# Strassen's token split of the second FFN moved from inside a 512-token tile to two whole tiles

## The chip, the cores and the metric

One core of a Trainium2 chip runs the whole program. The metric is the device time of one execution in microseconds (us). The profile is that of one execution, taken by the hardware profiler.

## The reference, cut to what is computed

```python
out = chunked_attention(q, k, v, mem_k, mem_v)   # 4 x 8 heads x 768 x 64
x = out.transpose(0, 2, 1, 3).reshape(3072, 512)
# first FFN
h = x @ w_in1                    # 512 -> 2048
g = s * relu(h) ** 2 + b
x = g @ w_out1                   # 2048 -> 512
# second FFN, the part that is changed
h = x @ w_in2                    # 512 -> 2048
g = h / (1 + exp(-1.702 * h))
out = g @ w_out2                 # 2048 -> 512
```

All is float32 outside. Inside, each operand of a matmul is split in two float32r parts, hi (a rounded copy) and lo (the rest), and each product is three matmuls: hi\*hi, hi\*lo, lo\*hi.

## The kernel before

There is one instruction stream per engine, in an order written out by hand, tied by semaphores; SyncE (SP) issues the DMAs. The first 58% of the span is attention together with the first FFN, in seven token tiles (M0 = 7, the last four of 480 tokens). The change does not touch it but for the last of these tiles, beside which the operands of the second FFN are prepared.

The second FFN runs in six tiles of 512 tokens. Its first product, w_in2 transposed times x, is done by Strassen's algorithm with seven products in place of eight. The rows of hidden features are taken in pairs of 128-row blocks (PAIRS = 8 pairs to a tile, so 48 turns `q`), the 512 input features in two halves of 256, and the tokens of a tile in two halves of 256 (HALF). One turn is seven products (`product`, L844 to L878), each of six matmuls with 256 columns: two of 128 input features, by three for hi and lo. Each goes to one of four PSUM banks. The seven weight sums (A11 to S4) of a pair are made once, for all eight pairs, and stay in `weights` for the whole stage; the seven token sums (B11 to T4) are made once per tile.

VectorE (DVE) puts the products together (`add_u2`, `add_u4`, `add_c12`, `add_c11`, `add_u3`, `add_c22`, `add_c21`, L1333 to L1366, each 128x256 from a PSUM bank and an SBUF tile). The four quadrants c11, c12 (even row block, two token halves) and c21, c22 (odd row block) form `h_even` and `h_odd`, each 128x512. ScalarE (ACT) copies the first product out (`keep_a11b11` L1080) and computes the sigmoids (`sigmoid_even` L1087, `sigmoid_odd` L1093); DVE multiplies (`gate_even` L1370, `gate_odd` L1374); ACT writes the hi part (`split_g2_hi` L1098) and DVE the lo part (`split_g2_lo` L1378) of what the second product eats.

The second product (`second_piece`, L813) takes one 128-row block f of the hidden features of one tile: four pieces (128 tokens each), each three matmuls with 512 columns, summed over f = 0 to 15 in the four banks `acc`. TensorE (PE) has the pieces of the pair before between the seven products: product, piece, product, piece, and at the end two pieces on end (L917 to L934). w_out2 comes anew for each tile, one 128-row block at a time: DMA (L449), hi by ACT (`split_w_out2_hi` L1055), lo by GpSimd (POOL, `split_w_out2_lo` L573) into a ring of four places.

Also beside this: `sum_rows` (POOL, L580 to L586) makes the weight sums of a pair, `split_rows_hi` (ACT, L1061) and `split_rows_lo` (DVE, L1324) split them, in one part of 128x1024 and one of 128x768; `sum_x2` (POOL, L591 to L598), `split_x2_hi` (ACT, L1074) and `split_x2_lo` (DVE, L1331) do the same with the tokens. `copy_result` (ACT L1109, DVE L1390) empties the four `acc` banks. Six of the eight weight pairs are made beside the last tile of the first FFN (steps of `ROWS_STEPS`), two in the second stage.

What a product waits for: the first of a turn for c11 of the turn before (and, in the first tile, for the weights of its pair), the second for u3, the third for c22, the fourth for c21, all of the turn before; the sixth for u2 and the seventh for c12 of its own turn. A second piece waits for hi and lo of its row block and for its w_out2 parts, and at f = 0 for the copies of the bank that it starts anew.

## Time and profile before

| what | value |
|---|---|
| three executions, median (lowest to highest) | 1205.45 us (1204.02 to 1214.04) |
| the profiled execution, its own time | 1205.65 us |
| its span in the profile | 1203.8 us |
| mean granted TensorE clock | 0.999 |
| PE busy / weight load busy | 99% / 89% |
| DVE / ACT / POOL busy | 63% / 55% / 30% |

The own time of an execution holds about 1.9 us around the span. A busy share is over the whole span; matmuls are pipelined and a recorded matmul is longer than the distance to the next one, so the cost of a matmul is read from the starts of successive ones. An instruction of DVE or ACT is likewise recorded somewhat longer than it keeps its engine from the next. "L876" is line 876 of the kernel before.

### The profile page before, as it was taken

To read this page: it belongs to the slowest core of one execution; us is meant where nothing else is said; L and a number is where in the kernel's file an instruction comes from. 1 tells how busy PE (TensorE), PEld (TensorE's weight loads), DVE (VectorE), ACT (ScalarE), POOL (GpSimd) and SP (SyncE) were. 2 spreads that over 40 slices of the span, in tenths; PEclk is the share of its full clock that TensorE was granted. 3 is DMA by queue.
4 is the path that set the end of the run, shared out by engine and by line. 5 is a ranking of instruction groups with operands and counts; after the bars stand their busy time and mean duration, and the time that the engine had idled before them with its cause. 6 is when DMAs were issued, how large, how long until landed. Compare 5 with 4: busy or idle time off the path is not lost. (4 is left out here: it accounts for less than half of the span.)

```text
span 1203.8 us, 21708 instructions
## 1 busy us (share of the span) xinstructions
PE 1190.3 (99%) x7224; PEld 1075.9 (89%) x7224; DVE 763.1 (63%) x2307; ACT 656.5 (55%) x1897; POOL 365.4 (30%) x364
## 2 busy tenths in 40 slices
PE   8899999999999999999999999999999999999998
PEld 5799999999888888888888889999999999999997
DVE  6788766777666666676536566655655656656554
ACT  6788666777666666666534444434433434444333
POOL 3775212222121121212015432422424224224221
PEclk9999999999999999999999999999999999999999
DMA  6752311321311311130021231231321311411211
GB/s 139 166 141 72 75 32 40 65 45 40 60 40 34 70 37 40 25 74 17 2 96 60 64 128 53 56 121 36 104 72 53 124 53 36 131 45 53 88 53 54
DMA packets 135637, 81.10 MB, mean 67 GB/s; under 512 B 95079, under 2 KB 115047, under 8 KB 135527
## 3 DMA queue, kind: packets, MB, share of 16 engines
q1 hardware_dynamic: 134304, 79.48, 25.2%
q8 instruction: 60, 0.98, 0.3%
q14 instruction: 50, 0.41, 0.1%
q10 hardware_dynamic: 1223, 0.23, 0.1%
HBM read 67.11 MB, written 12.58 MB: 66 GB/s over the span
## 5 line engine op out<-in xcount | busy, mean ns | idle before, releaser
L876 PEld LDWEIGHTS psum<-arena,weights 128*128 128x128 f32 x2016 | 285.6, 188 | 30.1 <-DVE arena_raw L1347 0.9
L808 PE MATMUL psum<-arena,weights 128*128 128x480 f32 (+1 forms) x1344 | 305.2, 366 | 0.2 <-DVE ffn L1311 0.2
L876 PE MATMUL psum<-arena,weights 128*128 128x256 f32 x2016 | 293.4, 281 | 0.5 <-DVE arena_raw L1347 0.5
L834 PE MATMUL psum<-g_hi,weights 128*128 128x480 f32 (+1 forms) x896 | 259.0, 363 | 0.1
L808 PEld LDWEIGHTS psum<-arena,weights 128*128 128x128 f32 x1344 | 237.8, 188 | 18.9 <-DVE ffn L1311 0.4
L832 PE MATMUL psum<-weights,g_hi 128*128 128x512 f32 x768 | 242.0, 396 | 0.1
L573 POOL TENSOR_TENSOR weights<-ffn,weights 128x512 fp32r<-128x512 f32 x94 | 129.4, 1396 | 327.8 <-ACT weights L1055 327.8
L834 PEld LDWEIGHTS psum<-g_hi,weights 128*128 128x128 f32 x896 | 164.5, 188 | 13.8 <-DVE g_lo L1317 0.4
L618 POOL TENSOR_TENSOR arena_raw<-arena_raw,small 96x256 f32<-96x256 f32 x96 | 58.6, 610 | 370.9 <-DVE small L1275 370.9
L834 PE MATMUL psum<-g_lo,weights 128*128 128x480 f32 (+1 forms) x448 | 163.4, 365 | 0.0
L832 PE MATMUL psum<-weights,g_lo 128*128 128x512 f32 x384 | 149.4, 389 | 0.0
L1255 DVE TENSOR_TENSOR arena<-psum,arena 128x96 fp32r<-128x96 f32 x336 | 83.2, 275 | 86.3 <-ACT arena L987 83.9
L832 PEld LDWEIGHTS psum<-weights,g_hi 128*128 128x128 f32 x768 | 122.3, 190 | 5.2 <-DVE g_lo L1378 0.3
L1087 ACT ACTIVATE arena_raw<-arena_raw 128x512 f32<-128x512 f32 x48 | 30.3, 632 | 164.2 <-issue 155.5
L992 ACT ACTIVATE arena_raw<-arena_raw,small 96x128 f32<-96x128 f32 x224 | 87.7, 392 | 35.1 <-DVE small L1264 34.9
L1317 DVE SCALAR_TENSOR_TENSOR g_lo<-ffn,columns,g_hi 128x480 fp32r<-128x480 f32 (+1 forms) x112 | 84.9, 758 | 29.1 <-ACT g_hi L1039 27.8
L1039 ACT ACTIVATE g_hi<-ffn,columns 128x480 fp32r<-128x480 f32 (+1 forms) x112 | 73.8, 659 | 45.2 <-PE psum L834 30.9
L1010 ACT ACTIVATE arena<-psum 64x96 fp32r<-64x96 f32 x224 | 54.7, 244 | 74.9 <-PE psum L751 70.5
L834 PEld LDWEIGHTS psum<-g_lo,weights 128*128 128x128 f32 x448 | 84.2, 188 | 6.4
L1378 DVE TENSOR_TENSOR g_lo<-arena_raw,g_hi 128x512 fp32r<-128x512 f32 x96 | 68.1, 710 | 33.9 <-ACT g_hi L1098 33.3
L832 PEld LDWEIGHTS psum<-weights,g_lo 128*128 128x128 f32 x384 | 72.2, 188 | 16.0
L1311 DVE SCALAR_TENSOR_TENSOR ffn<-psum,columns,ffn 128x480 f32<-128x480 f32 (+1 forms) x112 | 75.2, 671 | 15.3 <-ACT ffn L1031 10.9
(102 smaller groups left out, 1602.5 us busy)
## 6 DMA issues: line engine op xcount, KB each, us to landing
ffn<-in_moe_w_out_dram SPq DMA_DIRECT2D x94, 256.0 KB, 2.8
arena_raw<-in_k_dram SPq DMA_DIRECT2D x31, 240.0 KB
arena_raw<-in_v_dram SPq DMA_DIRECT2D x30, 240.0 KB
arena_raw<-x_scratch SPq DMA_DIRECT2D x6, 1024.0 KB, 5.6
arena_raw<-in_q_dram SPq DMA_DIRECT2D x31, 192.0 KB
out_dram<-result SPq DMA_DIRECT2D x5, 1024.0 KB, 4.5
result<-in_moe_w_out_dram SPq DMA_DIRECT2D x18, 256.0 KB, 3.0
result<-in_moe_w_in_dram SPq DMA_DIRECT2D x16, 256.0 KB, 3.1
```

The source lines that it names most:

```text
L573: nc.gpsimd.tensor_tensor(lo, w_out_raw(k), hi.bitcast(F32), ALU.subtract).then_inc(w_out2_ready, 1)
L618: nc.gpsimd.tensor_tensor(probs[:, n % 2, :, :], probs[:, n % 2, :, :], inv_total[:, n % 2, :].unsqueeze(2).to_broadcast([QT, 2, P]), ALU.mult
L808: last = nc.tensor.matmul(dst, w[:, kt * P:(kt + 1) * P], x, start=(kt + i == 0), stop=(kt == KT - 1 and i == 2))
L832: last = nc.tensor.matmul(acc[c][:, :], g[:, f % 2, piece], w, start=start, stop=stop)
L834: last = nc.tensor.matmul(acc[c][:, 0:n], w[:, piece], g[:, f % 2, 0:n], start=start, stop=stop)
L876: last = nc.tensor.matmul(bank_of[bank][:, 0:HALF], w[:, k * P:(k + 1) * P], x[:, k, :], start=(k + t == 0), stop=(k == 1 and t == 2))
L992: nc.scalar.activation(probs[:, n % 2, h, :], probs[:, n % 2, h, :], ACT.Exp, scale=-1.0, bias=exp_bias[:, n % 2, h:h + 1], accum_out=tota ...
L1039: nc.scalar.activation(g_hi[:, f % 2, 0:n], gated[:, 0:n], ACT.Identity, bias=b_col[:, 0:1]).then_inc(g_hi_done, 1)
L1255: last = nc.vector.tensor_tensor(qk_lo[parts, n % 2, cols], bank_qk[parts, source], qk_hi[parts, n % 2, cols].bitcast(F32), ALU.subtract)
L1311: nc.vector.scalar_tensor_tensor(out=gated[:, 0:n], in0=hid[f % 2][:, 0:n], scalar=s_col[:, 0:1], in1=nonlin[:, 0:n], op0=ALU.mult, op1=AL ...
L1317: nc.vector.scalar_tensor_tensor(out=g_lo[:, f % 2, 0:n], in0=gated[:, 0:n], scalar=b_col[:, 0:1], in1=g_hi[:, f % 2, 0:n].bitcast(F32), o ...
L1378: nc.vector.tensor_tensor(g_lo[:, e, :], (h_even, h_odd)[e], g_hi[:, e, :].bitcast(F32), ALU.subtract).then_inc(g_ready, 1)
```

## The change

A turn now covers two whole 512-token tiles, so that each of Strassen's products has 512 columns in place of 256. The second FFN has three blocks (BLOCKS = 3) of two tiles, 24 turns in place of 48. Of the four quadrants, c12 and c22 are those of the block's first tile (the "now" tile) and are used at once, as before; c11 and c21 are those of its second tile (the "later" tile), and are gated in place and kept in SBUF in float32 (`stored(f)`, 16 tiles of 128x512). After the eight turns of a block, PE has a stretch of second products alone: the last two row blocks of the now tile, and 14 of the later tile; its last two go between the products of the next block's first turn.

To make room, the weight sums do not stay: w_in2 is loaded, summed and split in each of the 24 turns, into two places in turn. The order of the token sums and who makes them change (T1 and T3 by POOL, T2 and T4 by DVE). For the later tile's row blocks, DVE makes the lo part of w_out2 in place of POOL. The raw tiles of w_out2 and the g tiles have four places in place of two.

The core of the diff:

```diff
-        def x2_parts(i, t):
+        def x2_parts(t):
+            pair, half = divmod(X2_ORDER.index(t), 2)
+            both = weights[:, pair, half * 2048:(half + 1) * 2048].rearrange("p (a k t) -> p a k t", a=2, k=2)
+        def rows_part(q, low, a):
+            first = (low * 7 + a) * HALF
+            return weights[:, 4 + q % 2, first:first + HALF]
+        def stored(f):
+            return weights_raw[:, 6 + f // 8, f % 8 * BT:(f % 8 + 1) * BT]
...
# SP
             def load_w_out2(k):
+                if k >= RING:
+                    sp.wait_ge(*w_out2_parts_made(k - RING))
-            def load_rows(p):
+            def load_rows(q):
+                p = q % PAIRS
+                if q:
+                    sp.wait_ge(rows_ready, q)
...
+            load_rows(1)
+            for s2 in range(BLOCKS):
+                for r in range(PAIRS):
+                    pair = PAIRS * s2 + r
+                    load_w_out2(turn(s2, 0, 2 * r + 2))
+                    load_w_out2(turn(s2, 0, 2 * r + 3))
+                    if r == 1:
+                        store_result(M0 + 2 * s2 - 1)
+                    if pair + 2 < PAIRS * BLOCKS:
+                        load_rows(pair + 2)
+                    if r == 2 and s2 + 1 < BLOCKS:
+                        load_x2(s2 + 1)
+                for f in range(NF):
+                    if turn(s2, 1, f + 2) < NF * 2 * BLOCKS:
+                        load_w_out2(turn(s2, 1, f + 2))
+                    if f == 2:
+                        store_result(M0 + 2 * s2)
...
# POOL
+            sum_rows(1)
+            for s2 in range(BLOCKS):
+                for r in range(PAIRS):
+                    q = PAIRS * s2 + r
+                    if q:
+                        split_w_out2_lo(turn(s2, 0, 2 * r))
+                        split_w_out2_lo(turn(s2, 0, 2 * r + 1))
+                    if r == 4 and s2 + 1 < BLOCKS:
+                        sum_x2(s2 + 1)
+                    if q + 2 < PAIRS * BLOCKS:
+                        sum_rows(q + 2)
...
# PE
-                        last = nc.tensor.matmul(bank_of[bank][:, 0:HALF], w[:, k * P:(k + 1) * P], x[:, k, :],
+                        last = nc.tensor.matmul(bank_of[bank][:, :], w[:, k * P:(k + 1) * P], x[:, k, :],
...
-            for q in range(PAIRS * M2):
+            for s2 in range(BLOCKS):
+                for r in range(PAIRS):
+                    q = PAIRS * s2 + r
+                    mm, f = (M0 + 2 * s2, 2 * r - 2) if r else (M0 + 2 * s2 - 1, NF - 2)
...
+                second_product(M0 + 2 * s2, NF - 2)
+                second_product(M0 + 2 * s2, NF - 1)
+                for f in range(NF - 2):
+                    second_product(M0 + 2 * s2 + 1, f)
...
# ACT
+            for s2 in range(BLOCKS):
+                for r in range(PAIRS):
+                    pair = PAIRS * s2 + r
+                    if r:
+                        split_now_hi(pair - 1, 1)
+                        sigmoid_c21(pair - 1)
+                    keep_a11b11(pair)
+                    if r == 1:
+                        copy_result(M0 + 2 * s2 - 1, 2)
+                    if pair:
+                        split_w_out2_hi(turn(s2, 0, 2 * r))
+                        split_w_out2_hi(turn(s2, 0, 2 * r + 1))
+                    if pair + 1 < PAIRS * BLOCKS:
+                        split_rows_hi(pair + 1)
+                    sigmoid_c12(pair)
+                    split_now_hi(pair, 0)
+                    sigmoid_c11(pair)
+                    if r == 0:
+                        copy_result(M0 + 2 * s2 - 1, 0)
+                    sigmoid_c22(pair)
+                split_now_hi(PAIRS * s2 + PAIRS - 1, 1)
+                sigmoid_c21(PAIRS * s2 + PAIRS - 1)
+                for f in range(NF):
+                    split_w_out2_hi(turn(s2, 1, f))
+                    split_later_hi(s2, f)
+                    if f == 2:
+                        copy_result(M0 + 2 * s2, 0)
+                        copy_result(M0 + 2 * s2, 2)
+                    if f in X2_HI and s2 + 1 < BLOCKS:
+                        split_x2_hi(s2 + 1, X2_HI[f])
...
# DVE
+            for s2 in range(BLOCKS):
+                for r in range(PAIRS):
+                    q = PAIRS * s2 + r
+                    if r:
+                        gate_c22(q - 1)
+                        split_g2_lo(turn(s2, 0, 2 * r - 1), h_odd)
+                        gate_c21(q - 1)
+                    if r == 1:
+                        copy_result(M0 + 2 * s2 - 1, 3)
+                    add_u2(q)
+                    if q + 1 < PAIRS * BLOCKS:
+                        split_rows_lo(q + 1)
+                    add_u4(q)
+                    add_c12(q)
+                    gate_c12(q)
+                    add_c11(q)
+                    split_g2_lo(turn(s2, 0, 2 * r), h_even)
+                    gate_c11(q)
+                    add_u3(q)
+                    add_c22(q)
+                    if r == 0:
+                        copy_result(M0 + 2 * s2 - 1, 1)
+                    add_c21(q)
+                gate_c22(PAIRS * s2 + PAIRS - 1)
+                split_g2_lo(turn(s2, 0, NF - 1), h_odd)
+                gate_c21(PAIRS * s2 + PAIRS - 1)
+                for f in range(NF):
+                    split_w_out2_lo(turn(s2, 1, f))
+                    split_g2_lo(turn(s2, 1, f), stored(f))
+                    if f in (1, 2):
+                        copy_result(M0 + 2 * s2, 2 * f - 1)
+                    if s2 + 1 < BLOCKS:
+                        if f in X2_LO:
+                            split_x2_lo(s2 + 1, X2_LO[f])
+                        if f in X2_SUMS:
+                            sum_x2(s2 + 1, X2_SUMS[f])
```

Beside the last tile of the first FFN, the new kernel makes the seven token sums of block 0 (each part 128x1024, twice the size of before), the weight sums of pair 0, and the first two row blocks of w_out2. Then `split_rows_hi(q)` waits until all seven products of turn q - 2 are done.

## Rows read from the trace of the kernel before

**Rows 1.** The page: busy time by engine, the chain's shares by line.

```profile
PE 1190.3 (99%) x7224; PEld 1075.9 (89%) x7224; DVE 763.1 (63%) x2307; ACT 656.5 (55%) x1897; POOL 365.4 (30%) x364
...
PE psum L832 22%; PE psum L876 19%; DVE weights L1324 0%; ACT weights L1061 0%; ACT arena_raw L1087 0%; DVE g_lo L1378 0%; ACT result L1109 0%; ACT weights L1055 0%; DVE arena_raw L1358 0%; DVE arena_raw L1362 0%; DVE arena_raw L1347 0%; DVE arena_raw L1370 0%
```

**Rows 2.** Busy time of stretches: first FFN's last tile, second FFN's steady part.

```profile
607.00:688.00 81.00, 81.00 (x375) 70.02 (x374) 44.51 (x52) 34.83 (x54) 29.86 (x30) 1.00 0.24 75
719.42:1193.72 474.30, 474.30 (x2971) 427.67 (x2971) 275.06 (x543) 198.39 (x362) 152.49 (x110) 1.00 0.23 70
```

**Rows 3.** Timeline of PE: start us, us, engine, line, what, xcount.

```profile
688.13 0.88 PE L876 MATMUL psum<-arena,weights 128*128 128x256 f32 x6
...
904.05 0.87 PE L876 MATMUL psum<-arena,weights 128*128 128x256 f32 x6
904.76 0.63 PE L832 MATMUL psum<-weights,g_hi 128*128 128x512 f32 x2
...
908.98 0.63 PE L832 MATMUL psum<-weights,g_hi 128*128 128x512 f32 x2
...
910.36 0.88 PE L876 MATMUL psum<-arena,weights 128*128 128x256 f32 x6
...
1194.94 0.61 PE L832 MATMUL psum<-weights,g_hi 128*128 128x512 f32 x2
...
1200.16 0.39 PE L832 MATMUL psum<-weights,g_lo 128*128 128x512 f32 x1
```

**Rows 4.** Timeline of DVE and ACT; in brackets idle before, and releaser.

```profile
783.06 0.69 DVE L1390 COPY result<-psum 128x512 f32<-128x512 f32 x1
...
907.53 0.69 DVE L1370 TENSOR_TENSOR arena_raw<-arena_raw 128x512 f32<-128x512 f32 x1 [0.75 <-ACT arena_raw L1087]
908.14 0.42 DVE L1358 TENSOR_TENSOR arena_raw<-psum,arena_raw 128x256 f32<-128x256 f32 x1
908.60 0.42 DVE L1362 TENSOR_TENSOR arena_raw<-psum,arena_raw 128x256 f32<-128x256 f32 x1
...
911.56 0.62 ACT L1098 ACTIVATE g_hi<-arena_raw 128x512 fp32r<-128x512 f32 x1
912.08 0.62 ACT L1074 ACTIVATE arena<-arena_raw 128x512 fp32r<-128x512 f32 x1
```

**Rows 5.** Timeline of ACT and DVE: one pair's weight sums are split.

```profile
681.98 1.79 ACT L1061 ACTIVATE weights<-arena_raw 128x1024 fp32r<-128x1024 f32 x2 [3.31 <-POOL arena_raw L586]
...
683.08 2.09 DVE L1324 TENSOR_TENSOR weights<-arena_raw,weights 128x1024 fp32r<-128x1024 f32 x2 [3.35 <-ACT weights L1061]
...
685.09 0.71 DVE L1311 SCALAR_TENSOR_TENSOR ffn<-psum,columns,ffn 128x480 f32<-128x480 f32 x1
```

**Rows 6.** Timeline of POOL beside DVE, where both read SBUF.

```profile
702.65 2.56 POOL L573 TENSOR_TENSOR weights<-ffn,weights 128x512 fp32r<-128x512 f32 x2 [9.77 <-ACT weights L1055]
...
704.08 3.08 DVE L1324 TENSOR_TENSOR weights<-arena_raw,weights 128x1024 fp32r<-128x1024 f32 x2 [0.44 <-ACT weights L1061]
...
713.65 0.74 POOL L586 TENSOR_TENSOR arena_raw<-arena_raw 128x256 f32<-128x256 f32 x1
713.66 1.27 DVE L1378 TENSOR_TENSOR g_lo<-arena_raw,g_hi 128x512 fp32r<-128x512 f32 x1 [0.70 <-ACT g_hi L1098]
714.35 3.00 POOL L573 TENSOR_TENSOR weights<-ffn,weights 128x512 fp32r<-128x512 f32 x2
...
715.38 0.42 DVE L1342 TENSOR_TENSOR arena_raw<-psum,arena_raw 128x256 f32<-128x256 f32 x1
```

**Rows 7.** A weight load and its use; POOL's 128x512 group after 690 us.

```profile
707.18 0.93 SPq L460 DMA_DIRECT2D arena_raw<-in_moe_w_in_dram  x2
710.86 0.74 POOL L580 TENSOR_TENSOR arena_raw<-arena_raw 128x256 f32<-128x256 f32 x1 [5.66 <-DMA arena_raw<-in_moe_w_in_dram]
L591 POOL TENSOR_TENSOR arena_raw<-arena_raw 128x512 f32<-128x512 f32 x5 | 6.5, 1291 | 0.0
```

**Rows 8.** PE's timeline: a stall in this stage.

```profile
707.54 0.98 PE L876 MATMUL psum<-arena,weights 128*128 128x256 f32 x6 [0.46 <-DVE arena_raw L1347]
```

More of the change, by code:

```diff
@@ L46 @@
 USES = {t: 1 + [x[1] for x in PRODUCTS].index(t) for t in range(7)}
+X2_ORDER = (B22, B21, B11, T1, T3, T2, T4)
+X2_NTH = {t: 1 + X2_ORDER.index(t) for t in range(7)}
 PAIRS = NF // 2
@@ L198, in bass_chunked_attention_two_ffn @@
-        h_even = raw_area(XSLOT + 9216, 512)
-        h_odd = raw_area(XSLOT + 9728, 512)
-        nonlin2 = raw_area(XSLOT + 10240, 512)
-        kept_a11b11, u2, u3 = (raw_area(3072 + i * HALF, HALF) for i in range(3))
-        def rows_raw(p):
-            return raw_area(0 if p >= PAIRS - 2 else XSLOT + 9216, 7 * HALF)
-        def w_out_raw(k):
-            return result[:, k * DM:(k + 1) * DM] if k < 2 else ffn[:, k % 2, :]
-        def raw_of(t):
-            k, half = {B11: (0, 0), T1: (0, 0), T3: (0, 1), B21: (2, 0), T4: (2, 0), B22: (2, 1), T2: (2, 1)}[t]
-            return x2_raw[:, k:k + 2, half * HALF:(half + 1) * HALF]
@@ L216, in rows_lo, with rows_parts @@
-        def rows_lo(p, a):
-            return weights[:, p, LOW + a * HALF:LOW + (a + 1) * HALF]
-        def rows_hi(p, a):
-            return weights[:, p, HIGH + a * HALF:HIGH + (a + 1) * HALF]
-        def ring(k):
-            return (weights[:, k % RING * 2 + a, REST:REST + DM] for a in range(2))
+        def rows_part(q, low, a):
+            first = (low * 7 + a) * HALF
+            return weights[:, 4 + q % 2, first:first + HALF]
+        def rows_parts(q, low):
+            return weights[:, 4 + q % 2, low * 7 * HALF:(low + 1) * 7 * HALF]
@@ new lines, in ring @@
+        def ring(k):
+            slot = k % RING
+            if slot < 2:
+                return (weights[:, 3, 2048 + (2 * slot + a) * DM:2048 + (2 * slot + a + 1) * DM] for a in range(2))
+            if slot == 2:
+                return (weights[:, 4 + a, 14 * HALF:14 * HALF + DM] for a in range(2))
+            return (area(2560 + a * DM, DM) for a in range(2))
+        def stored(f):
+            return weights_raw[:, 6 + f // 8, f % 8 * BT:(f % 8 + 1) * BT]
+        kept_a11b11, u2, u3, h_even, h_odd = (raw_area(i * BT, BT) for i in range(5))
@@ L227, in bass_chunked_attention_two_ffn, with raw_of @@
+        def raw_of(i, t):
+            if t == T1:
+                return (ffn if i else nonlin2.rearrange("p (k t) -> p k t", k=2))[:, :, :]
+            k, half = {B11: (0, 1), T3: (0, 0), B21: (2, 1), T4: (2, 1), B22: (2, 0), T2: (2, 0)}[t]
+            return x2_raw[:, k:k + 2, half * BT:(half + 1) * BT]
         q_raw = attn[0:QT, 0:2 * DM].rearrange("p (a c) -> p a c", a=2)
@@ L464, in load_x2 @@
             def load_x2(i):
-                if i == 0:
-                    sp.wait_ge(hid_ready, NF * (M0 - 1) + 1)
-                else:
+                if i:
                     sp.wait_ge(x2_ready, 7 * i)
-                first = start_of(M0 + i)
-                last = first + size_of(M0 + i)
+                first, last = 2 * BT * i, 2 * BT * (i + 1)
                 sp.wait_ge(result_stored, 16 * (1 + min(m for m in range(M0) if start_of(m) + size_of(m) >= last)))
@@ L1060, in split_rows_hi @@
                 for these in (slice(0, 4 * HALF), slice(4 * HALF, 7 * HALF)):
-                    nc.scalar.activation(weights[:, p, HIGH:REST][:, these], rows_raw(p)[:, these], ACT.Copy
+                    nc.scalar.activation(rows_parts(q, 0)[:, these], rows_raw[:, these], ACT.Copy
                                          ).then_inc(rows_hi_done, 1)
             def split_x2_hi(i, t):
-                if t < T2:
+                if t in (T1, T3):
+                    act.wait_ge(x2_first_summed, 2 * i + (1 if t == T1 else 2))
+                elif t in (T2, T4):
+                    act.wait_ge(x2_last_summed, 2 * i + (1 if t == T2 else 2))
+                else:
```

397 lines of the change are left out of this document (186 added, 211 removed).

## The prediction

> **What bounds the kernel now.** I read the page's busy times and chain first, then busy time by stretch, then the timelines of PE, of DVE and ACT, and of POOL beside DVE. The page puts the whole chain of the second stage on PE: the second product (L832) and Strassen's products (L876) hold 22% and 19% of the span, everything else next to nothing [rows 1]. By stretch, PE is busy 474.30 us of 474.30 in the steady part of this stage, and 81.00 of 81.00 beside the last tile of the first FFN, while DVE has 275 us and ACT 198 us of the 474 [rows 2]. So PE's own pace is the bound, and the question is what the change does to that pace, and whether the other engines, which get longer instructions with fewer gaps, can still follow.
>
> PE's pace comes from starts in its timeline. A product of six 256-column matmuls takes 904.05 to 904.76, 0.71 us, 0.1185 each; two pieces of together six 512-column matmuls take 908.98 to 910.36, 1.38 us, 0.2305 each; in the last stretch, of second products alone, 23 matmuls take 1194.94 to 1200.16, 0.227 each [rows 3]. The stage begins at 688.13 and its last matmul ends at 1200.55 [rows 3]: 512.4 us. Its floor is 2016 x 0.1185 + 1152 x 0.2305 + 24 of 480 columns (5.2, taken by width) = 509.6; the rest is small stalls like the 0.46 us at 707.54 [rows 8] and rounding.
>
> **The change part by part.** *PE.* 2016 matmuls of 256 columns become 24 x 7 x 6 = 1008 of 512. The trace has no 512-column matmul inside a product; the nearest rows give 0.227 to 0.2305 [rows 3]. I take 0.229: 230.8 us, where the half-size ones cost 2016 x 0.1185 = 238.9. Half of the second product's 1152 matmuls, some 600, now run without products between them, as in the last stretch, at about 0.2275: 136.5 us; the other 552 at 0.231 cost 127.5; plus 5.2. PE's new floor is 500.0 us, 12.4 below the 512.4 of now (bounds 497.7 to 503.8, with 0.227 or 0.2305 throughout). So twice the width halves the number of matmuls but hardly their total time: the most that can be won is about 1%.
>
> A rule bears on this. The trace has 0.1185 us for 256 columns, where the columns at 2.4 GHz (granted clock 1.00 [rows 2]) would take 0.107, so some 0.012 us per matmul goes with the count. The Trainium skill, TensorE: Matmul & The Clock Gate, section "Wait — 56ns, not 53.3ns?", states a fixed 2.5 ns on top of the columns; by it the products would shrink by only 2.6 us in place of 8.1. The trace's distances are larger, and the sum goes by them.
>
> *DVE and ACT in a turn.* A turn of PE is now 42 x 0.229 + 24 x 0.2308 = 15.16 us. The durations at twice the width: a 128x512 instruction of DVE that reads PSUM takes 0.69 us, as does one on SBUF, and the next starts 0.61 later; one that needs the result of the one ahead starts 0.04 after that one's end (908.14 + 0.42 to 908.60) [rows 4], so 0.73 after its start. ACT takes 0.62 and lets the next start after 0.52 [rows 4]. The two hi parts of a pair's weight sums take 1.79 us on ACT (about 1.05 for the wider), the two lo parts keep DVE from 683.08 to 685.09, 2.02 [rows 5]; these now come in every turn. Along the new order they close a ring, each step ending later than the step of PE that it also waits for:
> hi of the wider part, 1.09 with handoff; both lo parts on DVE, 2.02 (u4 stands behind them in DVE's queue); u4 0.73, c12 0.73, sigmoid 0.67, gate 0.60, c11 0.73, sigmoid 0.67, gate 0.60, u3 0.73, c22 0.73, sigmoid 0.67, gate 0.73: 7.59; then on ACT hi of the row block 0.52, sigmoid of c21 0.54, the copy of A11B11 0.52 and two hi parts of w_out2 1.04, all ahead of the next weight sums in its queue: 2.62. Sum 13.32 us, 1.84 below PE's turn.
>
> *The port.* POOL's share grows: the four weight sums (4 x 0.74 [rows 6], with gaps 3.2 us) in each of 24 turns, beside two lo parts of w_out2 (2.56 [rows 6]), so 5.8 us in 15.2. Where both work on SBUF, the one that comes second waits for the other's whole instruction: the weights' lo parts took 3.08 in place of 2.09 when they began 0.1 us into POOL's second instruction (702.65 + 1.28), and a 0.69 us instruction took 1.27 next to a POOL one begun 0.01 earlier; then POOL's pair took 3.00 in place of 2.56, and DVE's addition out of PSUM at 715.38 was not held [rows 6]. The Trainium skill, SBUF — State Buffer, section "Who interferes with whom", has this as an exclusive lock for the whole instruction, taken where DVE reads both inputs from SBUF; the trace agrees, and it speaks against the change.
> In the new order the w_out2 parts of POOL start just when the weights' hi parts are done: DVE finds the port held by the first or second of them, 1.1 us. The gate of c11 falls among the weight sums of the next pair, whose load takes 3.7 us from issue to use (707.18 to 710.86 [rows 7]) after the lo parts: 0.73, and the gate of c22 0.23. With these 2.06 us the ring is 15.38, against 15.16 of PE. Per turn that costs 0.2 us, and only once the slack with which a block starts (DVE has caught up in the stretch without products) is used up. The port waits can be anything from 0 to about 4 a turn, so the ring is 13.3 to 17.3; I take 15.4.
>
> *sum_x2 on POOL*, at turn 4 of blocks 0 and 1, is two instructions of twice 128x512. One 128x512 takes 1.29 [rows 7], so 2.45 each. They stand behind the w_out2 parts, and the second half of DVE's lo parts finds the port taken: it starts 2.45 us late, u4 and c12 with it, and the seventh product waits for c12. Walking the queues of this turn with the durations above, c12 is there at 14.1 us of the turn where PE asks at 12.1: a stall of 2.0 us in block 0. Turns 5 to 7 have nothing to spare and add 0.2 to 0.5 each, 1.0 together. In block 1 the same walk begins with more slack: 0.4, then 0.9. Block 2 has no such sum and I get no stall in its turns.
>
> *The end of a block* (0 and 1). The now tile's last row block, c22 of turn 7, is wanted after the two last pieces and one second product, 15.2 + 2.7 = 18.0 us into the turn. u3 comes at 16.6 as DVE is late by then; c22, c21, sigmoid, gate (with port), hi and lo take till 21.0: 3.0 us. The bank copies of ACT, which stand behind hi parts held up by this, come 0.7 late. Twice 3.7 = 7.4. In block 2, DVE is on time (u3 at 12) and both vanish. All stalls: 3.0 + 1.3 + 7.4 + 0.5 of smaller ones = 12.2 us.
>
> *The stretch without products.* 14 second products of 12 x 0.2275 = 2.73 us. DVE has 1.2 us for each (w_out2 lo and g lo), plus 9 instructions of 1.15 for the next tokens: 30 us of 44; ACT 1.04 each plus seven of 1.05. Four places in each ring let both run ahead. Cost 0; POOL is nearly idle here, so no port waits. *Loads.* 16 more loads of a pair's weights (512 KB each) go past SP in each turn with 10 us to spare, on DMA queues that moved 70 GB/s on average [rows 2]; cost 0, cover the 15 us turn. *Beside the last tile of the first FFN*, five weight pairs fewer and token parts of twice the size on engines that have 45 and 35 us of work in 81 [rows 2]; cost 0, up to 2 us if a POOL instruction holds a g part. *The kernel's end* is unchanged.
>
> **Sum.** 500.0 + 12.2 = 512.2 us for the stage, 0.2 less than the 512.4 of now. The profiled execution took 1205.65 us, 0.2 above the median of the three runs: 1205.4, and as a median 1205.
>
> **Rivals.** *PE stays the bound.* If the port waits are about 1 us a turn, the ring stays under 15.16 and sum_x2 and the block ends cost 2 to 3 us in all: stage 502.5, time 1195.7. For it: DVE lost nothing where it came first, as its 0.7 us instructions mostly do now, and 0.2 us of the ring decide. Against it: the order puts POOL's parts just ahead of DVE's largest instructions, and two POOL instructions on end leave no gap.
> *The ring decides, slower.* If each of some nine handoffs of the ring between engines takes 0.08 more than the 0.04 that I took, the ring is 16.1; with 3.5 us of port waits a turn it is 16.8. With 16.1, the same walk gives 26.8 us of stalls, a stage of 526.8, time 1220: 2 us for each 0.1 beyond 15.4. It is slower by over 1% from a ring of about 16.0 on. For it: ring and PE are within 2%, everything in the ring is in series, and DVE's busy share rises from 58% to over 70% in the turns. Against it: it takes handoffs of three times the length, or a third more port time.
> *That nothing of the width is won*, because 512 columns in a product cost 0.237: stage 520, time 1213, inside the forecast's side; the rows at 0.2305 speak against it.
>
> **How the numbers follow.** My forecast, a ring within 0.4 us of PE's turn, 0.64; PE bound 0.17; the ring decides 0.17; no width gain 0.02. A measurement of this kernel tells about 1% (12 us) from no change. Under 1193.4 only the lower half of the PE case lies, with a floor near 498: 0.10. Over 1217.5 lies most of the slower case: 0.15. The rest, 0.75, is within 1%. The range of 8 in 10 is 1195 (PE bound) to 1219 (ring of 16.1).
>
> **What would show it.** Right: product matmuls 0.229 apart; PE idle at the seventh product of turns 4 to 7 waiting for c12 (DVE), 2.0 us once and tenths after; 3 us at the second last row block of the now tile in blocks 0 and 1 waiting for g lo; block 2's turns at 15.2; DVE's weight lo parts over 3 us beside POOL. Wrong: turns of 15.2 everywhere, or 16 and more from turn 2 on, or PE waiting for weight loads or w_out2 parts, or the stage's floor off 500 by more than 4.

## The result and the profile after

The changed kernel takes 1190.44 us (median of five, 1190.09 to 1192.11) against 1205.45: a ratio of 0.9879, 95% interval 0.9848 to 0.9911. That is faster by 1.2%. The forecast was 1205 with a range of 1195 to 1219, and it was wrong; the rival "PE stays the bound" (1195.7) is what happened, though with port waits of 1.6 us a turn and not the "about 1" that it asked for, and even its time was 5 us too long.

The page of the kernel after, its busy times and its chain, which answer to [rows 1] (products are L910 now, second products L867):

```profile
PE 1172.3 (99%) x6216; PEld 1023.1 (86%) x6216; DVE 835.5 (70%) x2204; ACT 674.9 (57%) x1884; POOL 335.2 (28%) x362
...
PE 82%; DVE 6%; ACT 6%; issue 4%; POOL 1%; ACTq 0%; DVEq 0%; POOLq 0%
PE psum L869 21%; PE psum L842 20%; PE psum L867 18%; PE psum L910 13%; PE psum L785 3%; PE psum L809 3%; PE psum L796 2%; DVE weights L1404 1%; PE psum L773 1%; PE psum L772 1%; ACT weights L1101 1%; ACT weights L1111 1%; ACT arena_raw L1033 1%; PE psum L707 1%; ACT arena L1020 1%
```

PE is still the chain, and DVE has gone from 63% to 70%. The 6% of DVE and of ACT are no sign of the change, though. The chain of before was followed back only to 703 us, that of after through attention too; and in a second execution of this kernel (after_again, below), whose stage is as long to 0.05 us, PE holds 490 of the chain's last 500 us, where it holds 371 here. How short waits are shared out on the chain differs from one execution to the next, so what PE loses is read from the distances between its matmuls. Busy time by stretch, second stage (685.14 to 1185), answers to [rows 2]:

```profile
685.14:1185.00 499.86, 496.23 (x2185) 409.43 (x2183) 378.99 (x487) 237.50 (x385) 150.27 (x138) 1.00 0.30 93
```

PE is idle for 3.6 us by this count. From the stage's first matmul (685.14) to its last matmul's start (1184.69) it is 499.55 us; before it was 688.13 to 1200.16, 512.03. So 12.5 us came from the stage. The stage also began 3.0 us earlier, and that has nothing to do with the change. The first 60 us of four executions show it, in this order: after, before, before run once more, after run once more. The columns are PE, weight load, DVE, ACT and POOL busy, granted clock, DMA share, GB/s:

```profile
0.00:60.00 60.00, 52.95 (x406) 41.73 (x406) 42.34 (x196) 43.58 (x161) 35.05 (x39) 1.00 0.78 158
```
```profile
0.00:60.00 60.00, 52.30 (x387) 40.47 (x388) 40.70 (x189) 40.70 (x151) 31.90 (x36) 0.97 0.70 152
```
```profile
0.00:60.00 60.00, 53.20 (x404) 42.10 (x405) 42.28 (x195) 43.36 (x160) 34.75 (x38) 1.00 0.72 157
```
```profile
0.00:60.00 60.00, 53.67 (x337) 41.42 (x338) 34.56 (x163) 33.88 (x126) 26.77 (x31) 0.74 0.61 132
```

The granted clock at the start was 1.00, 0.97, 1.00 and 0.74, and the stage then began at 685.1, 688.1, 685.5 and 696.8 us. In the last of these the clock was at its lower level (1.2 GHz) from about 15 to 45 us, while PE was busy; the row is after run once more:

```profile
20.00:25.00 5.00, 5.00 (x31) 3.87 (x32) 2.94 (x14) 3.09 (x14) 2.27 (x2) 0.50 0.24 54
```

One program differs from itself by nearly 12 us before the stage begins, so in what follows kernels are compared by the stage alone, from its first matmul to the start of its last.

PE's timeline, turn 4 of block 0 and the end of block 0, answers to [rows 3]. The last column is the idle time before and what ended it:

```profile
746.93 1.52 PE L910 MATMUL psum<-weights 128*128 128x512 f32 x6
748.29 0.84 PE L867 MATMUL psum<-weights,arena 128*128 128x512 f32 x3
748.97 1.52 PE L910 MATMUL psum<-weights 128*128 128x512 f32 x6
...
804.73 2.88 PE L867 MATMUL psum<-weights,arena 128*128 128x512 f32 x12
808.88 3.02 PE L867 MATMUL psum<-arena 128*128 128x512 f32 x12 [1.26 <-DVE arena L1486]
812.37 0.70 PE L867 MATMUL psum<-weights,g_hi 128*128 128x512 f32 x2 [0.47 <-ACT result L1184]
```

A product takes 1.36 us and a piece 0.68: nine matmuls in 2.04 us, 0.2267 each, products and pieces alike. No turn of PE has a stall: the starts of all turns stand 14.96 us apart (66 x 0.2267), the first of the stage 14.88. What stalls there are stand at the ends of blocks 0 and 1, by the distances between matmuls 1.42 and 0.63 in block 0, 1.62 and 0.60 in block 1, and 0.19 in each block for the matmul just behind them: 4.66 us. PE's floor in the stage is then 494.9 us.

DVE and POOL in turn 4 of block 0 (from 744.89), where the forecast had its 2.0 us, answer to [rows 5, 6]:

```profile
749.40 5.28 DVE L1404 TENSOR_TENSOR weights<-arena_raw,weights 128x1024 fp32r<-128x1024 f32 x2 [0.22 <-ACT weights L1111]
754.60 0.68 DVE L1440 TENSOR_TENSOR arena_raw<-psum,arena_raw 128x512 f32<-128x512 f32 x1
755.38 0.69 DVE L1445 TENSOR_TENSOR arena_raw<-psum,arena_raw 128x512 f32<-128x512 f32 x1
```
```profile
747.97 2.55 POOL L606 TENSOR_TENSOR weights<-arena_raw,weights 128x512 fp32r<-128x512 f32 x2 [2.81 <-ACT weights L1101]
750.48 3.38 POOL L627 TENSOR_TENSOR ffn<-arena_raw 128x1024 f32<-128x1024 f32 x1
```

Both lo parts meet POOL, as forecast: first its w_out2 lo part, then the first x2 sum, and 2.08 us of work (the same pair in turn 0, alone) takes 5.28. But c12 (L1445) is written at 756.07, 11.2 us into the turn. The forecast had 14.1, and PE asks at 12.2.

### The profile page after: what moved, and what is told of

It reads as the page before. It is cut to its first block, busy times and chain, and to the rows that moved or that the text cites. A ratio compares the mean times of both kernels' runs of the same rounds, so it can differ in the third digit from the quotient of the medians.

```text
span 1188.3 us, 19471 instructions
## 1 busy us (share of the span) xinstructions
PE 1172.3 (99%) x6216; PEld 1023.1 (86%) x6216; DVE 835.5 (70%) x2204; ACT 674.9 (57%) x1884; POOL 335.2 (28%) x362
## 4 chain that ended last, share of the span: by engine, by line
PE 82%; DVE 6%; ACT 6%; issue 4%; POOL 1%; ACTq 0%; DVEq 0%; POOLq 0%
PE psum L869 21%; PE psum L842 20%; PE psum L867 18%; PE psum L910 13%; PE psum L785 3%; PE psum L809 3%; PE psum L796 2%; DVE weights L1404 1%; PE psum L773 1%; PE psum L772 1%; ACT weights L1101 1%; ACT weights L1111 1%; ACT arena_raw L1033 1%; PE psum L707 1%; ACT arena L1020 1%
## 5 line engine op out<-in xcount | busy, mean ns | idle before, releaser
L910 PE MATMUL psum<-weights 128*128 128x512 f32 x1008 | 255.9, 389 | 0.0
L842 PEld LDWEIGHTS psum<-arena,weights 128*128 128x128 f32 x1344 | 237.7, 188 | 18.9 <-DVE ffn L1391 0.4
L910 PEld LDWEIGHTS psum<-weights 128*128 128x128 f32 x1008 | 189.2, 188 | 39.2
L867 PE MATMUL psum<-weights,g_hi 128*128 128x512 f32 x384 | 118.4, 390 | 0.9 <-ACT result L1184 0.9
L606 POOL TENSOR_TENSOR weights<-arena_raw,weights 128x512 fp32r<-128x512 f32 x36 | 46.3, 1298 | 217.8 <-ACT weights L1101 217.8
L1072 ACT ACTIVATE ffn<-psum 128x480 f32<-128x480 f32 (+1 forms) x112 | 60.0, 536 | 52.1 <-PE psum L842 51.7
L867 PEld LDWEIGHTS psum<-weights,g_hi 128*128 128x128 f32 x384 | 71.9, 188 | 16.6 <-DVE g_lo L1486 1.7
L1020 ACT ACTIVATE arena<-psum 128x96 fp32r<-128x96 f32 x336 | 75.6, 259 | 16.9 <-PE psum L773 14.1
L1404 DVE TENSOR_TENSOR weights<-arena_raw,weights 128x1024 fp32r<-128x1024 f32 (+1 forms) x48 | 76.3, 1628 | 12.1 <-ACT weights L1111 12.1
L1344 DVE CUSTOM_DVE_ANT_0 arena_raw<-psum,masks 96x128 f32<-96x128 f32 x224 | 55.4, 283 | 36.0 <-ACT arena L1051 35.6
```

What stands on the lines that cost most here:

```text
L842: last = nc.tensor.matmul(dst, w[:, kt * P:(kt + 1) * P], x, start=(kt + i == 0), stop=(kt == KT - 1 and i == 2))
L867: last = nc.tensor.matmul(acc[c][:, :], g[:, piece], w, start=start, stop=stop)
L910: last = nc.tensor.matmul(bank_of[bank][:, :], w[:, k * P:(k + 1) * P], x[:, k, :], start=(k + t == 0), stop=(k == 1 and t == 2))
L1020: last = nc.scalar.activation(qk_hi[parts, n % 2, cols], bank_qk[parts, source], ACT.Copy)
L1072: nc.scalar.activation(nonlin[:, 0:n], hid[f % 2][:, 0:n], ACT.Relu).then_inc(nonlin_done, 1)
L1404: last = nc.vector.tensor_tensor(rows_parts(q, 1)[:, these], rows_raw[:, these], rows_parts(q, 0)[:, these].bitcast(F32), ALU.subtract)
```

## The experiments

Edits are against the kernel after, unless said. "Lag" is how far into PE's turn ACT begins the hi parts of the next pair's weight sums (L1111); in the kernel after it is 3.67 in turn 1, falls by 0.08 a turn to 3.43 in turn 4, jumps to 5.57 in turn 5 behind the x2 sums and is 5.40 in turn 7.

**before_again.** The kernel before, once more.

> The kernel before, unchanged, for a second profile. The changed kernel was 3.0 us ahead already when the second FFN began (685.1 us in place of 688.1), all of it gained in the first 49 us, where both programs are the same. If that lead is an accident of one profile (loads that land sooner or later), this profile starts the second FFN somewhere between 684 and 689 us and its stage takes 512.4 us again. If the change itself gives the lead, it starts at 688.1 again.

Measured: 1202.96 us. The stage begins at 685.53 (688.13 in the profile of before, 685.14 after) and takes 512.03 us, the same to 0.01. So the stage's lengths can be compared to hundredths, and 2.6 of the 3.0 us before the stage are the start's own.

**after_again.** The kernel after, once more. Expected was a stage of 499.55 us again, within 0.1, and 1190 to 1192 us for executions with a mean clock of 1.000; the rival was that the change itself makes the start 3.0 us faster.

Measured: 1191.68 us as a median of six (ratio 0.9897, 0.9856 to 0.9938); the three with a mean clock of 1.000 took 1190.6 to 1191.3, the profiled one with 0.987 took 1201.78. Its stage is 499.60 us, with the same stalls at the ends of blocks (1.51 and 0.60, 1.58 and 0.64).

**split256.** Each product as twelve matmuls of 256 columns, `half` being the first and then the second 256, all else as changed:

```diff
-                        last = nc.tensor.matmul(bank_of[bank][:, :], w[:, k * P:(k + 1) * P], x[:, k, :],
+                            last = nc.tensor.matmul(bank_of[bank][:, half], w[:, k * P:(k + 1) * P], x[:, k, half],
```

> The changed kernel with each 512-column matmul of a product issued as two of 256 columns; everything else is as changed. Theory pace: what was won is TensorE's time per column. 256-column matmuls stand 0.118 us apart, 512-column ones 0.2267, and the second product's matmuls between short ones 0.2305. A turn is then 84 x 0.118 + 24 x 0.2305 = 15.47 us in place of 14.96, 12.2 us more over 24 turns, of which up to 4 come back since the other engines now have slack: 1198 to 1203 us. Theory structure: what was won is fewer and longer steps and fewer waits: then this stays at 1190 to 1192 us.

Measured: 1206.23 us (ratio 0.9993, 0.9955 to 1.0032); stage 509.29 us without a single stall, turns 15.58. The median of the times says little: five of the ten executions had the low clock at the start (0.987 to 0.989; 1209.8 to 1211.7 us), the other five took 1199.9 to 1202.7.

```profile
731.96 1.59 PE L911 MATMUL psum<-weights 128*128 128x256 f32 x12
733.39 0.86 PE L867 MATMUL psum<-weights,arena 128*128 128x512 f32 x3
734.09 1.59 PE L911 MATMUL psum<-weights 128*128 128x256 f32 x12
```

Twelve halves take 1.43 us where six whole ones take 1.36, and three pieces 0.70 where they take 0.68. The gain is PE's own and comes from the width: without it the stage is 9.7 us longer, and against PE's floor of 494.9 the width gives 14.4, of which the stalls take 4.7. All the rest of the change gives 2.7 us (512.03 to 509.29). With a slower PE there are also no stalls.

**ladder.** Five of the six matmuls of each product cut to 64, 128, 192, 240, 256, 272, 320 and 416 columns in turns 0 to 7 of a block (this leaves out part of every product).

> The changed kernel with five of the six matmuls of each product cut to 64, 128, 192, 240, 256, 272, 320 and 416 columns in turns 0 to 7 of a block (so most of the hidden features are left out of the sums); the trace gives the distance of matmuls at each width. Theory issue: a matmul with its weight load cannot follow the last one sooner than some 0.118 us: distances stay at 0.118 from 64 to 256 columns, are 0.120 at 272 and 0.142 at 320, and the 512-column matmul after the short ones stands 0.233 from the next. Theory fixed cost: each matmul costs its columns at 2.4 GHz and about 0.012 us more: 0.039, 0.065, 0.092, 0.112, 0.118, 0.125, 0.145, 0.185.

Measured, the median distance from one such matmul to the next between neighbours of its own width: 111, 112, 113, 112 ns for 64 to 240 columns, then 120 (256), 125 (272), 147 (320), 189 (416), 216 (480, from the first FFN) and 227 (512). Two rows of turn 0:

```profile
686.69 0.86 PE L911 MATMUL psum<-weights 128*128 128x512 f32 x6
687.39 0.68 PE L869 MATMUL psum<-g_hi,weights 128*128 128x480 f32 x2
```

One matmul of 512 and five of 64 columns take 0.70 us, hardly less than six of 256 took before (0.71 [rows 3]): up to 240 columns a matmul between others as narrow costs 0.112 us, however narrow it is. Above, 256 and 512 columns fit one line of 0.0042 us per 10 columns and about 0.013 per matmul (0.120 and 0.227). The ladder gives no reading of the loop's own length, as the short turns let DVE and ACT fall behind.

**ring_plus.** Two more 128x256 copies on ACT in each turn, ahead of the w_out2 hi parts.

> The changed kernel with two more 128x256 copies on ScalarE in each turn (into a place that nothing reads), ahead of the two hi parts of w_out2. Theory ring: the ring of waits between ScalarE and VectorE takes 14.88 us in the changed kernel, 0.08 below TensorE's turn; with 0.56 more it is 15.44, which is what was predicted. c12 has 3.0 us to spare in turn 1, loses 0.48 a turn and 2.2 by sum_x2 in turn 4: stalls of 0.7 in turn 4, 0.5 in turns 5 to 7 and 1.1 more at the end of the block, 3.2 us in each of blocks 0 and 1, next to none in block 2: 6 to 7 us slower, 1197 us. Theory hidden: ScalarE is busy 57% and the copies cost nothing: 1190 to 1191 us.

Measured: 1197.49 us (ratio 0.9957, 0.9928 to 0.9987), stage 505.03, 5.5 us more. The copies keep ACT for 0.60 us, but the lag grows by only 0.23 a turn where it fell by 0.08: 0.31. The other 0.29 comes off the wait for the port, since the lo parts now begin later in POOL's instruction (the pair takes 2.77 us, not 3.08). Until late in turn 4 PE feels nothing; its first stall is at that turn's seventh product, 0.43 us in block 0 and 0.81 in block 1. From turn 5 the lag is 7.0 and stops there, and PE waits instead. Block 2, where the lag only gets to 5.9, has no stall. Of the 5.5 us, 1.6 are matmuls at 1.2 GHz behind the stall at the end of block 0. What PE waits for is what the forecast named, only later and less:

```profile
PE psum L869 <- DVE arena L1493: 4.6, 2, 2.3
PE psum L912 <- DVE arena_raw L1452: 0.5, 1, 0.5
PE psum L869 <- ACT result L1191: 0.5, 1, 0.5
```

**rows_first.** ACT makes the hi parts of the weight sums ahead of the two w_out2 hi parts:

```diff
                     keep_a11b11(pair)
...
+                    if pair + 1 < PAIRS * BLOCKS:
+                        split_rows_hi(pair + 1)
                     if pair:
                         split_w_out2_hi(turn(s2, 0, 2 * r))
                         split_w_out2_hi(turn(s2, 0, 2 * r + 1))
-                    if pair + 1 < PAIRS * BLOCKS:
-                        split_rows_hi(pair + 1)
```

> The new kernel with one move on ACT: the two hi parts of the sums' weight rows go ahead of the two w_out2 hi parts. Theory (the stalls that are left, 4.66 us at the ends of blocks 0 and 1, come from a lag of the loop over ACT and DVE behind TensorE of about 5.4 us in turns 5 to 7, of which POOL's two x2 sums give 2.2 in turn 4): the hi parts begin about 1.0 us earlier behind TensorE's turn (3.5 to 2.5 us), the first weight lo part begins before POOL's w_out2 lo part and takes 1.2 us in place of 2.21, so the lag in turns 5 to 7 falls from 5.5 to 3 or 4 and the stalls at the block ends go from 4.66 us to under 1; the stage from 499.6 to about 495.5, the time 4 us under the new kernel's. Rival 1 (the lag has nothing to do with it: the block ends stall by their own chain of now rows and bank copies): the stage stays at 499.6 within 0.5. Rival 2 (POOL takes the port between the two lo parts, so that the second takes 2.2 in place of the first): the loop gains 1.0 us at most, the stalls fall by half, the stage is about 497.5.

Measured: 1186.94 us (ratio to before 0.9846, 0.9812 to 0.9879), stage 495.01, 4.5 us less. The lag is 2.1 in all turns but 1 (2.7 to 3.0), 5 (4.8) and 6 (2.9), and the stalls are 0.2 us in the whole stage. Rival 2 is right about the port and wrong about the result:

```profile
721.86 3.18 DVE L1404 TENSOR_TENSOR weights<-arena_raw,weights 128x1024 fp32r<-128x1024 f32 x2
```
```profile
722.13 4.06 POOL L606 TENSOR_TENSOR weights<-arena_raw,weights 128x512 fp32r<-128x512 f32 x2 [4.50 <-ACT weights L1101]
```

DVE comes first this time (721.86, POOL 722.13), POOL gets the port between the two lo parts, and the pair takes 3.18 us, no less than before. Now POOL waits too (4.06 in place of 2.55), off any path. What was won is the 1.0 us of w_out2 parts on ACT, which no longer stand in the loop.

**sumx2_gap.** POOL's two x2 sums in turns 4 and 5, each behind the lo parts of its turn:

```diff
-                    if r == 4 and s2 + 1 < BLOCKS:
-                        sum_x2(s2 + 1)
+                    if r in (4, 5) and s2 + 1 < BLOCKS:
+                        pool.wait_ge(rows_ready, q + 2)
+                        sum_x2(s2 + 1, r - 4)
```

> The new kernel with POOL's two x2 sums put into turns 4 and 5, each after the lo parts of the weight rows, where DVE has short operations only. Theory (the x2 sums hold the port under a weight lo part, 5.28 us for the pair of lo parts in turn 4 in place of 3.1, and that lag of 2.2 us lasts to the block's end and is what stalls TensorE there): the lag of the hi parts in turns 5 to 7 stays under 4.2 us in place of 5.4 to 5.7, both stalls of 1.4 to 1.6 us on a g_lo row go, the stage comes to about 495.5 and the time 4 us under the new kernel's. Rival (an x2 sum in the gap delays u4, c12 or a gate by its own 2.5 us, and these are what TensorE's next product waits for): stalls of 1 to 2 us move into turns 4 and 5, and the stage stays within 1 us of 499.6.

Measured: 1193.36 us as a median of four executions (ratio 0.9884, 0.9831 to 0.9937), of which two had the low clock at the start (0.989; 1196.7 and 1197.5) and two not (1188.5 and 1190.0), so the times alone do not tell it from the kernel after; stage 496.90, 2.65 us less. No stall in a turn. In block 0 the lag is 4.5 in turn 7 and 0.64 us of stall on the g_lo row are left; in block 1 it is 3.84 and there is none. The 0.6 to 0.7 us for a bank copy stays in both. The pair of lo parts takes 3.08 in turn 4 too. The jump of 2.2 us was thus the first x2 sum under the lo parts; about 0.8 in two turns is what the sums cost in the gap (c12's gate 0.94 in place of 0.69, and the weight sums behind them).

**both.** Meant as both moves together, but as run it had the hi parts of the weight sums one place further ahead, in front of the copy of A11B11 too.

> Both moves together. Theory: the loop of ACT and DVE is about 1 us a turn shorter than TensorE's turn of 14.96 and carries no lag to the block's end, so TensorE never waits in the stage: stage 494.9 (499.55 less the 4.66 us of stalls), time 4.7 us under the new kernel's. Rival (the ends of blocks have a chain of their own): at least 1.2 us (2 x 0.6, the waits for a bank copy) stay, stage 496.1 or more.

Measured: 1210.77 us (ratio 1.0041, 1.0013 to 1.0070), stage 519.23: turns of 14.96 to 15.14 us up to turn 3, then 16.1 to 17.1, in block 2 as well, where no x2 sum runs. ACT's timeline:

```profile
717.44 1.78 ACT L1114 ACTIVATE weights<-arena_raw 128x1024 fp32r<-128x1024 f32 x2
719.13 0.58 ACT L1135 ACTIVATE arena_raw<-psum 128x512 f32<-128x512 f32 x1
719.60 1.14 ACT L1104 ACTIVATE weights<-arena_raw 128x512 fp32r<-128x512 f32 x2
```

and DVE's:

```profile
719.80 0.69 DVE L1437 TENSOR_TENSOR arena_raw<-psum,arena_raw 128x512 f32<-128x512 f32 x1 [1.46 <-ACT arena_raw L1135]
720.41 4.23 DVE L1407 TENSOR_TENSOR weights<-arena_raw,weights 128x1024 fp32r<-128x1024 f32 x2
```

u2 (L1437) now waits for the copy, which stands behind the hi parts; the lo parts stand behind u2, each of the two meets one of POOL's parts, and the pair takes 4.2 us. The loop is about 16.4 us long: this is the forecast's slower rival, made real by one more place in ACT's queue.

**both2.** The two moves as they were meant, hi parts behind the copy.

> The hi parts of the sums' weight rows ahead of the two w_out2 hi parts, and behind the copy of A11B11 this time, with POOL's x2 sums in turns 4 and 5. Theory (the order of the copy and the hi parts cost the 24 us of the kernel in which the hi parts were ahead of both: u3 waited for the copy, the lo parts came late and both of them then met POOL's w_out2 parts): every turn 14.96 us, no stalls, stage 494.9 to 495.1, time equal to rows_first (1186.94) within 1 us. Rival (POOL's wait for the lo parts in turns 4 and 5 is what cost it, since the loads of the weights stand behind POOL): turns of 16.4 us from turn 4 on again, stage over 515.

Measured: 1186.76 us (ratio to before 0.9839, 0.9794 to 0.9884), stage 495.02, all turns 14.96. The order of the copy and the hi parts was the cause. POOL's wait alone is not, and brings nothing on top of rows_first, as there was no stall left to take.

**rows_first_plus.** rows_first with the two extra copies of ring_plus.

> rows_first with the two extra 128x256 copies of ACT in each turn, which cost the new kernel 5.5 us (stage 505.0 against 499.55). Theory (with the hi parts first the loop is over 0.6 us a turn shorter than TensorE's turn, so it has room for the copies): turns 14.96 us, stalls under 0.5 us in all, stage 495.0 to 495.5. Rival (the loop is at balance there too and the order only shifted its phase): the lag grows by 0.3 us a turn again, stage 497 or more.

Measured: stage 495.03, stalls 0.26 us, lag 2.1 again (one execution, 1193.8 us with a clock of 0.993 and a stage that began only at 693.4). Copies that cost the changed kernel 5.5 us cost nothing here. This shows that their place matters, and not how much room the loop has: they now stand behind the hi parts of the weight sums, where ACT waits 3.9 us for DVE in rows_first. What room there is shows in rows_first itself, where the lag falls from 4.8 to 2.9 us from turn 5 to turn 6, in a turn whose lo parts met no POOL part (2.09 us), while in the kernel after it falls by 0.08.

**late_start.** Three extra 128x512 copies on ACT, each waited for, behind the first sigmoid of the stage.

> The new kernel with three extra 128x512 copies on ACT, each waited for, behind the first sigmoid of the stage: ACT and DVE start the stage 2.0 us later behind TensorE, once, as the prediction had them. Theory (the loop of ACT and DVE takes 14.88 us a turn, TensorE 14.96, so a lag is kept and hardly worked off; TensorE stalls once the rows' hi parts begin over 7.0 us into its turn, as they did with two more copies a turn): in block 0 the hi parts begin at 5.6 us in turns 1 to 4 and at 7.0 in turn 5, where TensorE stalls for about 0.5 us, and at the end of block 0 the wait for a g_lo row grows from 1.4 to about 2.7 us; block 1 and block 2 as in the new kernel. Stage 501.2 us (499.55 + 0.5 + 1.3), up to 503 if the wait at the block's end lets the granted clock fall for some matmuls, as in the run with two more copies. Rival (the lag at a block's end comes from POOL and the port alone, and a late start is caught up within the turns): the hi parts are back at 3.5 us by turn 4, stage 499.6.

Measured: 1193.59 us (ratio 0.9906, 0.9871 to 0.9942), stage 501.46. The copies took 1.95 us, of which 1.0 arrived in the lag: 4.69 in turn 1, 4.46 in turn 4, 6.42 in turn 5, 6.23 in turn 7. It is kept, as said, and block 1 is as in the kernel after. At the seventh product of turn 4 PE stalls 0.14 us, at the end of block 0 2.24 where it was 1.42, and then:

```profile
800.00:809.00 9.00, 9.00 (x41) 7.27 (x39) 8.02 (x11) 2.47 (x4) 3.38 (x4) 1.00 0.39 117
811.00:816.20 5.20, 4.95 (x15) 3.95 (x16) 5.20 (x10) 5.20 (x10) 0.00 (x0) 0.67 0.21 54
816.20:820.00 3.80, 3.80 (x18) 3.13 (x17) 3.42 (x5) 3.08 (x6) 0.00 (x0) 1.00 0.63 213
```

PE goes on at 811.25, and from 813 to 816 its matmuls stand 0.427 us apart (granted clock 0.67 over the stretch of 5.2 us, that is 1.2 GHz for part of it): 1.6 us more, beside which the 0.7 for the bank copy is gone. So the stage met its forecast of 501.2 in part by luck: the lag and the stalls came out smaller (4.7 and 6.4 us, 0.14 and 0.8 more, where 5.6 and 7.0, 0.5 and 1.3 were expected), and the clock made up for it.

## Why the prediction was wrong, by its steps

The forecast was 15 us too long (1205.4 against 1190.4). By the profiles: PE's floor 4.9 (495.1 with the last matmul itself, as the forecast counted), stalls 7.5, the start 3.0. So two steps failed. The price of a 512-column matmul was drawn up towards rows of before whose neighbours are narrow (0.229 for the products, 0.231 for half of the pieces), though the row with neighbours as wide gave 0.227; all cost 0.2267. And the walk of the queues had ACT and DVE too late behind PE: a ring longer than PE's turn, and c12 2.9 us too late, which made 12.2 us of stalls where 4.66 were measured. The kinds of wait, at the ends of blocks and at the port, were right.

*The base, 1205.65.* It came from an execution whose clock was 0.97 in its first 60 us, 2.6 us later at the stage than before_again. The text called it 0.2 above the median, which is true and hid it: executions of this program with a mean clock of 1.000 take 1202.5 to 1204.1.

*PE's floor: 500.0, measured 494.9.* Two terms were mis-sized. The product matmuls were taken at 0.229 and cost 0.2267 (2.3 us). The pieces were taken at 0.231 between products and 0.2275 apart from them, and also cost 0.2267 (2.8 us). The row behind 0.2305 [rows 3] was read as the price of a piece. It is the price of a piece behind short matmuls: in before_again the three matmuls of a piece that follows 256-column ones cost 233, 236 and 228 ns (medians), against 227 where their neighbours are as wide. This goes away when the product is widened. split256 shows it from the other side: it keeps the 256 columns, and the same 233, 236 and 228 ns behind them, but has half as many crossings from short to wide (168, not 336). Its second products are 4.0 us shorter than those of before (273.2 to 269.2): 2.9 for the crossings at 17 ns each, 0.2 for pieces on end, some 0.9 for the stalls that before has. Its products are 1.3 us longer (238.8 to 240.1), which leaves the 2.7. So the 12.5 us are: 1008 for 2016 product matmuls 10.3 (238.8 less 228.5), crossings 5.8 (336 x 17.3 ns) and 0.5 of the same kind in second pieces on end, a stall of before 0.5 [rows 8], less 4.66 of new stalls: 12.4. The rule of the Trainium skill (TensorE: Matmul & The Clock Gate, "Wait — 56ns, not 53.3ns?"), 2.5 ns on top of the columns, is further off than the text had it: 256 and 512 columns both give about 13 ns, and the products shrank by 10.3 us, not 2.6 (1008 fewer matmuls at 2.5 ns are 2.5).

*The ring, 15.38 against 15.16.* The ring without port was right: 14.88 measured, less port waits of 1.6, is 13.3, and the text had 13.32. The port waits were sized 2.06; in the turns the wide lo part takes 2.21 in place of 1.2 (1.0), the gate of c11 1.23 in place of 0.69 (0.54), the gate of c22 0.76 (0.07). So the ring was 0.5 us shorter and PE's turn 0.2 us shorter than thought, and the order of the two turned round: 14.88 under 14.96 instead of 15.38 over 15.16. The text had said that 0.2 us of the ring decide.

*Stall at turn 4 (2.0 and 1.0; 0.4 and 0.9).* Measured: none. The mechanism was there in full, the lo parts at 5.28 us and a lag 2.2 us longer to the end of the block, but c12 came 11.2 us into the turn, not 14.1. Of the 2.9 us, 0.3 a turn for three turns is the ring, which was to add 0.2 and took off 0.08. The other 2 us are a remainder. The expectation of late_start puts them down to the start of the stage, where the walk would have had ACT and DVE that much too late. The prediction does not print where its walk began, so what made up the 2 us is not shown; one candidate of 1.28 us is ACT's table load, which in the trace falls into a wait:

```profile
687.19 1.78 ACT L1111 ACTIVATE weights<-arena_raw 128x1024 fp32r<-128x1024 f32 x2
688.99 1.28 ACT L1138 ACT_TABLE_LOAD   x1
693.53 0.63 ACT L1138 ACTIVATE arena_raw<-arena_raw 128x512 f32<-128x512 f32 x1 [3.26 <-DVE arena_raw L1445]
```

In the kernel before it had come late, at 695.00, behind a wait of 5.58 us for DVE. late_start and ring_plus put a part of the lag back (1.0 and 1.6 us in turn 4), and the stall at the seventh product returned, with 0.14 and 0.43 us in block 0.

*The ends of blocks, 2 x 3.7.* Place and kind were right (g lo of the now tile first, then the bank copies), the size was not: 4.66 in all. The size follows the lag: with a lag of 3.84, 4.5, 5.40, 5.58 and 6.23 us in turn 7 the stall on the g lo row was 0, 0.53, 1.42, 1.62 and 2.24 us, one for one above some 4.0. At a lag of 7.0 (ring_plus) it was 2.45 and 2.43, half a microsecond under that line. A walk 2 us late at the stage's start can account for block 0 only: late_start changed block 0 and left block 1 as it was. What made block 1's 3.7 too large (2.4 measured) is not parted by any run; a ring thought 0.3 us a turn too long works in that direction.

*Block 2, the stretch without products, loads, the last tile of the first FFN: 0.* Right; PE has no stall of note in any. The stage starts at 685.14 in after and at 685.53 in before_again; variants that are the same as after up to there start it between 685.2 and 686.5 with the same start clock of 1.00, so no effect of what lies ahead, the five weight pairs fewer among it, can be told from that scatter.

*The port* was right as a mechanism, in the trace and in four experiments: the waits are for the whole of the other engine's instruction, and an instruction that comes later waits less, to the tenth (ring_plus). The Trainium skill says the first too (SBUF — State Buffer, "Who interferes with whom"): the lock is exclusive, and whoever issues first has the shared ports for the whole instruction.

*The chances.* "Faster by over 1%" stood at 0.10 since the floor's lower bound had been 497.7. That bound was added up wrongly: 2160 matmuls at 0.227, "throughout", and 5.2 are 495.5 us, and the upper one at 0.2305 is 503.1, not 503.8. The floor measured by the same count, 495.1, lies just under the right lower bound, which was a row of the trace of before: the 23 matmuls whose neighbours are all as wide [rows 3]. With 495.5 the case "PE stays the bound" would have reached down to about 1191 us with its 2 to 3 us of stalls, and the chance of over 1% would have been larger.

## What to carry to other kernels

The distance between matmuls belongs to a pair of neighbours, not to a line of code: before pricing a change of width, sort the distances by the width of the matmul ahead and look what the change does to the neighbours, too. Where two loops are within a few per cent of each other, a lag that one event leaves stays for the rest of the block; so ask what cheap work stands in the longer loop for no reason. One such move on ACT took 4.5 us off the stage here, and with one place more it was 20 us longer than it had been. And price the start of the profiled execution against a second one before its time is taken as the base.

## What was unexpected of the hardware

- The granted clock in the first 60 us, a mean over stretches at 2.4 and 1.2 GHz, was 1.00, 0.97, 0.86, 0.77 or 0.74 in the thirteen profiles, and the stage then began at 685.1 to 686.5, 687.8 to 688.1, 693.4, 695.2 or 696.8 to 696.9 us. It goes with nearly all the spread of the times: of the 17 executions of the kernel before that ran beside both, the 11 with a mean clock of 1.000 took 1202.7 to 1204.1 us, one with 0.998 took 1205.0, and the five with 0.987 to 0.993 took 1210.3 to 1214.3.
- Up to 240 columns a float32r matmul with weights of its own costs 0.112 us between others of its width; 256 columns cost 0.120. Six halves of a product were thus close to where halving brings nothing.
- Matmuls of 512 columns behind 256-column ones are slower by 6, 9 and 1 ns, three in a row.
- A stall of 2.2 to 2.5 us of PE was followed, after a few matmuls, by some 3 us at 1.2 GHz in ring_plus, late_start and both, and one of 1.4 to 1.6 us was not. In ring_plus and in both, one stall of 2.4 to 2.5 us had this after it and another of the same length had not; what tells them apart is open.
